# Fused attention, two feed-forward layers and a Fourier mix: operand splits and transposes put into earlier gaps of the matmul order

## The reference

```python
# q, k, v: (2, 8, 768, 64); n_global = 8, n_local = 96
scores = q @ k^T / 8 + bias(distance), masked to the 8 global keys and a window of 96 behind each query
x = softmax(scores) @ v                      # then heads side by side: (2, 768, 512)
# first block: mix along the sequence, then a feed-forward layer
u = x + (x^T @ U @ V)^T                      # U (768, 32), V (32, 768)
x = u + relu(u @ w_ch1) @ w_ch2              # w_ch1 (512, 2048), w_ch2 (2048, 512)
# second block: Fourier mix, normalise, feed-forward layer
u = x + real(fft(fft(x, axis=1), axis=2))
un = (u - mean(u)) / sqrt(var(u) + 1e-6)     # over the 512 features
out = u + relu(un @ w_ch1') @ w_ch2'
```

## Time and profile before

| | before |
|---|---|
| median of 3 runs | 687.99 us (686.96 to 689.87) |
| the profiled execution | 689.87 us |
| its span, first to last instruction | 688.1 us |
| PE busy | 669.6 us, 97% |
| PEld busy | 600.5 us, 87% |
| DVE busy | 409.6 us, 60% |
| ACT busy | 330.4 us, 48% |
| POOL busy | 362.8 us, 53% |

### The profile page before, as it was taken

The page is one execution under the profiler, slowest core; times in us unless marked ns, Lnnn a source line. Parts: engine busy times, 40 slices in busy tenths (PEclk is TensorE's granted clock), DMA queues, the critical chain, the costliest instruction groups (busy, mean ns, idle before and its releaser), DMA issues.

```text
span 688.1 us, 10361 instructions
## 1 busy us (share of the span) xinstructions
PE 669.6 (97%) x3658; PEld 600.5 (87%) x3658; DVE 409.6 (60%) x930; ACT 330.4 (48%) x721; POOL 362.8 (53%) x375
## 2 busy tenths in 40 slices
PE   8999899999999999999999999999999999999998
PEld 6989789999899888888989988988898889889886
DVE  7555555555444557764587577564876664445454
ACT  4766556543334367443353476432444673443330
POOL 0401034435544699945555876445555965566611
PEclk9999989999999999999999999999999999999999
DMA  7442334112212431212111122122211122221232
GB/s 247 152 136 104 105 104 138 36 55 62 61 33 61 142 100 53 71 61 63 33 60 61 62 63 72 50 63 61 63 61 51 47 89 62 62 61 62 62 122 92
DMA packets 50532, 54.07 MB, mean 79 GB/s; under 512 B 4432, under 2 KB 37328, under 8 KB 50352
## 3 DMA queue, kind: packets, MB, share of 16 engines
q1 hardware_dynamic: 50480, 53.40, 24.5%
HBM read 53.39 MB, written 3.15 MB: 82 GB/s over the span
## 4 chain that ended last, share of the span: by engine, by line
PE 84%; DVE 6%; ACT 5%; POOL 2%; issue 2%; DVEq 0%; ACTq 0%; POOLq 0%
PE yP L760 12%; PE yP L762 12%; PE yP L761 11%; PE Yb L739 5%; PE Yb L741 5%; PE Yb L740 5%; PE aP L654 3%; PE aP L628 3%; PE Xb L739 3%; PE Zb L739 3%; PE Xb L740 3%; PE Zb L740 3%; PE Zb L741 3%; PE Xb L741 3%; ACT PB L892 1%
## 5 line engine op out<-in xcount | busy, mean ns | idle before, releaser
L519 POOL TENSOR_TENSOR WCL<-w_stage,WCH 128x512 fp32r<-128x512 f32 (+1 forms) x128 | 145.0, 1158 | 167.2 <-ACT WCH L977 167.2
L1297 DVE TENSOR_TENSOR Y<-yP,Y 128x512 f32<-128x512 f32 x192 | 129.5, 686 | 82.3 <-PE yP L762 81.8
L760 PE MATMUL yP<-WOH,hidH 128*128 128x512 f32 x384 | 152.7, 398 | 3.8 <-DVE Y L1297 3.5
L762 PE MATMUL yP<-WOH,hidL 128*128 128x512 f32 x384 | 151.5, 394 | 0.0
L761 PE MATMUL yP<-WOL,hidH 128*128 128x512 f32 x384 | 151.0, 393 | 0.0
L525 POOL TENSOR_TENSOR WOL<-o_stage,WOH 128x512 fp32r<-128x512 f32 x64 | 81.8, 1301 | 66.5 <-ACT WOH L984 66.5
L987 ACT ACTIVATE hidH<-Xb 128x384 fp32r<-128x384 f32 x64 | 31.4, 491 | 150.6 <-PE yP L762 150.6
L760 PEld LDWEIGHTS yP<-WOH,hidH 128*128 128x128 f32 x384 | 72.2, 188 | 20.1 <-DVE Y L1297 7.2
L762 PEld LDWEIGHTS yP<-WOH,hidL 128*128 128x128 f32 x384 | 72.0, 188 | 15.8
L761 PEld LDWEIGHTS yP<-WOL,hidH 128*128 128x128 f32 x384 | 72.1, 188 | 10.8
L739 PE MATMUL Yb<-UCH,WCH 128*128 128x384 f32 x192 | 65.3, 340 | 0.0
(11 more groups left out here) (214 smaller groups left out, 1299.2 us busy)
## 6 DMA issues: line engine op xcount, KB each, us to landing
w_stage<-w_in SPq DMA_DIRECT2D x128, 128.0 KB, 2.3
o_stage<-w_out SPq DMA_DIRECT2D x32, 512.0 KB, 3.4
V<-v_win SPq DMA_DIRECT2D x8, 704.0 KB, 6.6
K<-k_win SPq DMA_DIRECT2D x8, 644.0 KB, 5.3
Q<-q_t SPq DMA_DIRECT2D x16, 192.0 KB, 3.4
Y<-x_scratch SPq DMA_DIRECT2D x8, 384.0 KB
out<-Y SPq DMA_DIRECT2D x12, 256.0 KB, 3.6
CSraw<-seq_dft SPq DMA_DIRECT2D x1, 1348.0 KB, 5.6
```

The costliest lines, as they stand in the source:

```text
L519: nc.gpsimd.tensor_tensor(WCL[:, g % 2, u0:u1, :, :], w_stage[:, 1 + u0:1 + u1, :, :], hi32(WCH[:, g % 2, u0:u1, :, :]), ALU.subtract).the ...
L760: nc.tensor.matmul(bank[:, :], hh, WOH[:, h % 2, f, :], start=f == 0, stop=False)
L762: mm = nc.tensor.matmul(bank[:, :], hl, WOH[:, h % 2, f, :], start=False, stop=f == 1)
L1297: nc.vector.tensor_tensor(y, yP[t % 2][:, :], y, ALU.add).then_inc(s_yadd, 1)
```

## The change

Two tables of positions are edited; no operation is added, removed or altered.

```diff
-            for product, late in zip(PRODUCTS, (3, 5, 7, GAPS, GAPS + 3, GAPS + 5, GAPS + 7)):
+            for product, late in zip(PRODUCTS, (3, 5, 7, 8, GAPS + 2, GAPS + 4, GAPS + 6)):
                 put(GAPS * (g - 1) + late, "split_hi", c, product)
                 put(GAPS * (g - 1) + late + 1, "split_lo", c, product)
...
-            for n in range(22, 49):
+            for n in range(22, 48):
                 for i in range(HT):
-                    for late, *what in ((9, "turn", i, 0), (11, "turn", i, 1), (0, "dim", i, 0), (1, "dim", i, 1), (2, "combine", i, 0), (3, "stats", i, 0),
+                    for late, *what in ((8, "turn", i, 0), (10, "turn", i, 1), (0, "dim", i, 0), (1, "dim", i, 1), (2, "combine", i, 0), (3, "stats", i, 0),
```

## The result

| | before | after |
|---|---|---|
| median, us | 687.60 (686.96 to 689.87, 4 runs) | 695.31 (694.72 to 696.17, 4 runs) |
| the profiled execution, us | 689.87 | 696.75 |
| its span, us | 688.1 | 695.0 |

The ratio is 1.0109, with a 95% interval of 1.009 to 1.013: the change makes the kernel slower by 1.1%. The medians are 7.7 us apart, and the interval is 6.2 to 8.9. I had forecast 694.8 (691.0 to 698.0), and 696.7 for the profiled execution.

The account below looks back on a forecast made before the run. PE was taken as full where the change acts, so every wait of PE lengthens the result. Terms 3.8 + 0.5 + 1.7 + 0.8 = +6.8 us on the median of 687.99 gave 694.8 us, range 691.0 to 698.0.

Parts of the forecast that it names:

- P1 of round B, three times: At three operand changes, P2's split moved into round A makes P1 1.26 us later each; +3.8 us (2.8 to 4.5).
- P7, P4 and P3 in round B: Earlier splits in round B: L4 newly stalls 0.62, stalls of L5 and next P1 go; +0.5 us (-1.4 to 1.9).
- `turn` (0, 0), two entries: First `turn` of each entry, now directly behind L3: PE waits 0.87 us for UN each time; +1.7 us.
- the third `turn` by way of POOL, two entries: `turn` (2, 0) ahead of L2 delays ACT, POOL, then L5 of round A by 0.40 at rounds 16 and 24; +0.8 us.
- the other `turn`s: Remaining moved transposes only change place; 0 us, with 0.11 to spare at (1, 0) and about 0.1 at (2, 1).
- Rival 1: Losses half hidden: P2's split falls into ACT's and DVE's idle time, P1's part is 0; 691.0 us, chance 12%.
- The signs to look for: Idle time in the new profile: P1 1.3 to 1.5 us, L4 0.5 to 0.6, L837 0.8 to 0.9, L5 about 0.9.
- Rival 2: Not slower: P2's split over by 403.21, when L5's relu may start, so old stalls go; 686.6 us, chance 4%.
- Rival 3: UN waits out one more POOL operation, so two `turn`s (1, 0) stall; +2.5 us, 697.3 us, chance 8%.
- Rival 4: PE's clock falls after the new stall before P1 at the three changes; +5.2 us, 700 us, chance 4%.
- the whole prize: All there is to win, from the waits of L5 and P1 around the operand changes: near 3.1 us.
- Catching up: By the skill's rule PE, with weight loads at 87%, could win stalls back; the forecast rejected this and kept losses whole.

Follow-up runs that it names:

- e1: Only P2's operand split moved to gap 8 of round A, other splits and turns as in the kernel before; 693.22 us, ratio 1.0061.
- e2: Only the splits of P7, P4 and P3 moved one item forward in round B, against the kernel before; 689.47 us, ratio 1.001.
- e5: Only `turn` (0, 0) of each batch entry moved one calm gap earlier, against the kernel before; 686.93 us in one execution.
- e6: Only `turn` (2, 0) of each batch entry moved one calm gap earlier, against the kernel before; 691.95 us in one execution.
- e4: Against the kernel before, P2's high half moved early on ACT as in the change, its low half on DVE left in round B; 689.56 us, ratio 1.0007.
- e8: e7 plus the second fold's last part one gap later and its split two gaps later, in rounds 10 and 18; 682.32 us, ratio 0.9905 against the kernel before.
- e7: Against the kernel before, separate gaps for ACT's and DVE's split halves, low halves behind the additions they held up, turns unmoved; 686.73 us, ratio 0.9976.

## Why the prediction was right, and where it was off

| step | forecast | in the whole change, from the matmuls' starts | with that part alone |
|---|---|---|---|
| P1 of round B, three times | 3.8 | 1.29 + 1.29 + 1.28 = 3.86 | 3.81 (e1) |
| P7, P4 and P3 in round B | 0.5 | 0.12 + 0.18 + 0.12 = 0.42 | 0.71 (e2) |
| `turn` (0, 0), two entries | 1.7 | 0.85 + 0.87 = 1.72 | 1.68 (e5) |
| the third `turn` by way of POOL, two entries | 0.8 | 0.36 + 0.34 = 0.70 | 0.76 (e6) |
| the other `turn`s | 0 | 0 | |
| sum | 6.8 | 6.7 | |

- **P1.** The step held because it priced the place in DVE's queue, 1.02 of work and 0.24 of waiting for ACT, and the trace has 1.02 and 0.26. e4 confirms the split between the engines. Rival 1 had this loss hidden in idle time. It was right about ACT's part (0.15 is left of it when DVE's is taken away) and wrong about DVE's.
- **Round B.** The matmuls behind L4's stall come 0.61 later, for 0.62 expected. L5's stall gives back 0.31 to 0.32 and the next P1's 0.14 to 0.16, for 0.31 and 0.15. The net is a difference of these three, and its size is no better than the 0.1 by which the table is read: 0.42 for 0.5, and 0.71 where the part stands alone. The sign held in both. The bounds that the forecast gives for this part in its range should be -1.9 and +1.4, not -1.8 and +1.5; nothing hangs on it.
- **The first `turn`.** Its wait was plain from two rows of the trace before, the end of L3 and the start of UN.
- **The third `turn`.** The path over L2, ACT, POOL and ACT back to PE was found in the right place, and took 0.36 and 0.34 in the whole change, 0.39 and 0.37 alone, for 0.40.
- **The other `turn`s.** L837 has 0.19 of idle time in front at (1, 0) and 0.26 at (2, 1) of the profile after, where I had none (the second is the half that ACT's copy feeds, for which I had 0.1 to spare). Neither moves the matmuls behind it in the table of shifts.
- **The signs to look for.** P1's idle time of 1.47 and 1.48 lies in the 1.3 to 1.5 that were named. L4's 0.67 and L837's 1.12 and 1.14 are above the 0.5 to 0.6 and 0.8 to 0.9 named, and L5's 0.80 below the 0.9. For L4 and L837 I had named what PE loses, and the list shows the idle time of weight loads, which is another thing: 1.12 there was 0.86 on PE, 0.48 was 0.31, and 0.19 was 0.15 in front of P1 and nothing in front of `turn` (1, 0).
- **Rival 2** (not slower) fell at the place named for it: P2's split was not over when the relu could start: the relu's row at 406.84 has no idle time in front. **Rival 3:** UN at `turn` (1, 0) takes 1.59 (at 364.37), for 1.69 before, so it was not held up once more. Which operation of POOL holds it was not tried. **Rival 4:** over the two new stalls of round 16 the granted clock stays at 1.00:

```profile
404.00:424.00 20.00, 18.22 (x88) 15.80 (x89) 13.68 (x27) 13.44 (x25) 12.05 (x12) 1.00 0.21 62
```

- **What there was to win.** The 3.1 us that the forecast calls the whole prize are only what stood around the operand changes. e8 won 6.05, more than half of it at the two folds.
- **Catching up.** By the Trainium skill (Perfetto Trace Analysis, Identifying the Most-Contended Engine) the weight loads' share, 87%, would leave room to win back what a stall cost. This case's traces don't agree: the shifts never fall back by more than the 0.1 of their reading, and e5's 0.77 stays whole.

That the total came so near is partly luck. The small misses are of both signs, and the medians differ by 7.7 where the traces have 6.6: a median has its own microsecond.

## What to carry to other kernels

Where PE is full, price an operation that is moved by what it then stands in front of in its own engine's queue, and ask whether something on PE waits for that; free time of the engine elsewhere doesn't help. Work in two halves on two engines should get a place on each, right behind what PE waits for there, and not one place with a fixed distance. Moving a feeder earlier was worth nothing where no wait stood at its consumer. All that was won here had stood in the list of weight loads as a wait; what a wait costs is read from the matmuls' starts.

## What the runs showed of the hardware

The same program runs up to 6.9 us apart on one chip (the kernel before, 31 runs) and 8.2 us in e7, and most of the difference goes with TensorE's granted clock, averaged over an execution. The kernel before in the first comparison on one chip: 691.7 us at 0.990 (3 runs), 689.6 at 0.993 (10), 688.7 at 0.995 (8), 687.0 at 0.998 (7). The changed kernel, in all its recorded executions, has 696.2 at 0.993 (13 runs) and 695.4 at 0.995 (10). At equal clock the difference is 6.6 and 6.7, which is closer to the 6.6 of the traces than the medians' 7.7. Whether the two sets ran on the same chip isn't known.

The clock differs in the attention stage, which no experiment touched. The windows of the kernel before, and then of the kernel with the first `turn` moved, whose execution came to round 5 4.6 us sooner:

```profile
60.00:80.00 20.00, 18.34 (x132) 17.32 (x132) 9.83 (x37) 11.07 (x39) 2.96 (x3) 0.91 0.36 127
80.00:110.00 30.00, 26.88 (x170) 24.81 (x169) 16.61 (x56) 18.44 (x55) 7.72 (x9) 0.89 0.18 60
```

```profile
60.00:80.00 20.00, 18.15 (x142) 17.03 (x142) 10.65 (x39) 11.93 (x37) 2.95 (x3) 1.00 0.34 122
80.00:110.00 30.00, 25.82 (x184) 23.66 (x182) 19.67 (x68) 20.79 (x61) 10.20 (x11) 1.00 0.22 72
```

In the first the clock was for part of the stretch at 1.2 GHz in place of 2.4, in the second at 2.4 throughout. Why the one execution drops and the other doesn't stays open. Not all of a difference is the clock: 0.5 of the 4.6 us were there by 20 us, with the clock at 1.00 in both. In the kernel with `turn` (2, 0) moved PE was 2.2 us later than in the kernel before by that point, also at 1.00, and its 691.95 us stand 3.3 above the 688.6 of the kernel before on its chip at the same clock of 0.995 (5 runs), where its edit costs 0.7. What held up its first 20 us stays open. Stalls of PE of 1.2 to 1.4 us in the feed-forward rounds left the clock at 1.00, in the changed kernel and in e1.
